# Linear-attention state from five chunks of 115 and 116 rows instead of six of 96, a head's last row by a transfer of its own

## What is computed

```python
kv = einsum('bhsd,bhse->bhde', k, v)          # 8 batches, 8 heads, 576 rows, head size 64
out = einsum('bhsd,bhde->bhse', q, kv)
x = out / sqrt(mean(out * out) + 1e-6) * g_norm     # 4608 x 512
h = x @ w_in;  g = max(h, 0) + alpha * min(h, 0);  y = g @ w_out      # 512 -> 2048 -> 512
e = argmax(y @ w_gate);  out[token] = gate * relu(y @ w1[e]) @ w2[e]  # eight experts
```

## Time and profile before

| | us |
|---|---|
| median of 3 runs | 1503.25 |
| lowest, highest | 1499.38, 1505.24 |
| the profiled execution, its time | 1500.92 |
| the profiled execution, its span | 1499.1 |
| TensorE busy in it | 1468.6 |
| VectorE, ScalarE, GpSimd busy | 723.5, 491.3, 127.6 |

### The profile page before, as it was taken

One profiled execution on the slowest core, in us unless ns is written; L12 is line 12 of the kernel. 1 busy time (PEld: TensorE's weight loads), 2 busy tenths in 40 slices (PEclk: granted clock), 3 DMA queues, 4 the chain that ended last, 5 costly groups with the idle time before them and its releaser, 6 DMA issues.

```text
span 1499.1 us, 27268 instructions
## 1 busy us (share of the span) xinstructions
PE 1468.6 (98%) x8553; PEld 1277.5 (85%) x8554; DVE 723.5 (48%) x1796; ACT 491.3 (33%) x994; POOL 127.6 (9%) x143
## 2 busy tenths in 40 slices
PE   7899999999999999999999999999999999999997
PEld 6788989888898989898989898887888888888886
DVE  3585555565656465645555655663122114444411
ACT  3442232323232323223222221433233234444422
POOL 1000000000000000000000000112111111111111
PEclk8999999999999999999999999999999999999999
DMA  8532121102121102213100000524123114444410
GB/s 193 136 95 70 33 75 33 43 2 75 33 75 33 43 2 61 46 36 71 31 13 23 1 22 1 146 88 156 44 91 106 43 37 149 155 142 157 152 41 32
DMA packets 100516, 104.51 MB, mean 70 GB/s; under 512 B 55296, under 2 KB 75920, under 8 KB 100434
## 3 DMA queue, kind: packets, MB, share of 16 engines
q1 hardware_dynamic: 91618, 80.99, 19.6%
q0 software_dynamic: 7872, 21.09, 4.4%
q10 hardware_dynamic: 944, 1.33, 0.4%
HBM read 84.04 MB, written 20.65 MB: 70 GB/s over the span
## 4 chain that ended last, share of the span: by engine, by line
PE 90%; DMA 4%; DVE 2%; ACT 1%; issue 1%; SPq 1%; POOL 0%; ACTq 0%; POOLq 0%; DVEq 0%
PE psAcc L1346 25%; PE psH L1334 24%; PE psAcc L1469 15%; PE psH L1448 14%; PE psO L1458 2%; PE psO L1279 2%; PE psO L1249 1%; PE psQ L1429 1%; PE psQ L1265 1%; DMA AR<-rows,uid 1%; PE psY L1297 1%; DMA lists<-meta,slot 1%; PE psY L1289 1%; PE psY L1306 1%; DMA AR<-in_v_dram 1%
## 5 line engine op out<-in xcount | busy, mean ns | idle before, releaser
L1346 PE MATMUL psAcc<-W,XG 128*128 128x512 f32 x1728 | 438.9, 399 | 0.0
L1334 PE MATMUL psH<-XG,W 128*128 128x384 f32 x2304 | 436.3, 337 | 2.2 <-DVE W L958 1.4
L1334 PEld LDWEIGHTS psH<-XG,W 128*128 128x128 f32 x2304 | 408.4, 188 | 18.0 <-issue 2.7
L1346 PEld LDWEIGHTS psAcc<-W,XG 128*128 128x128 f32 x1728 | 313.7, 188 | 66.1 <-issue 6.0
L683 ACT ACTIVATE XG<-AR 128x128 fp32r<-128x128 f32 (+1 forms) x384 | 132.1, 364 | 639.9 <-DVE AR L988 634.2
L985 DVE TENSOR_SCALAR AR<-psH,acol 128x384 f32<-128x384 f32 x192 | 118.4, 617 | 296.0 <-PE psH L1334 296.0
L1448 PE MATMUL psH<-W,XG 128*128 (+1 forms) x996 | 250.4, 400 | 0.0
L1469 PE MATMUL psAcc<-W,XG 128*128 (+1 forms) x984 | 243.4, 396 | 0.0
L1469 PEld LDWEIGHTS psAcc<-W,XG 128*128 128x128 f32 x984 | 182.9, 189 | 37.3
L1448 PEld LDWEIGHTS psH<-W,XG 128*128 128x128 f32 x996 | 180.8, 188 | 36.8 <-DVE W L966 0.4
L1153 DVE TENSOR_TENSOR XG<-psO,XG 128x512 fp32r<-128x512 f32 x82 | 56.6, 690 | 222.1 <-ACT XG L742 218.8
(11 more groups left out here) (200 smaller groups left out, 873.3 us busy)
## 6 DMA issues: line engine op xcount, KB each, us to landing
AR<-in_moe_w_dram SPq DMA_DIRECT2D x68, 512.0 KB, 4.9
AR<-in_k_dram SPq DMA_DIRECT2D x16, 576.0 KB, 5.4
rows<-AR SPq DMA_DIRECT2D x36, 256.0 KB, 2.1
AR<-in_q_dram SPq DMA_DIRECT2D x32, 256.0 KB, 3.1
AR<-in_v_dram SPq DMA_DIRECT2D x14, 576.0 KB, 6.8
AR<-in_moe_w_in_dram SPq DMA_DIRECT2D x16, 256.0 KB, 2.9
AR<-in_moe_w_out_dram SPq DMA_DIRECT2D x16, 256.0 KB, 3.5
AR<-in_v_dram ACTq DMA_DIRECT2D x2, 576.0 KB, 9.3
```

What stands on the lines that cost most here:

```text
L1334: mm = pe.matmul(psH[f % 2][:, 0:TILE], w_in_v[:, wp, cc, f * P:(f + 1) * P], xT[:, b, xp, cc, :], start=(cc == 0 and (wp, xp) == PARTS[0] ...
L1346: mm = pe.matmul(psAcc[m][:, :], gT[:, f % 2, gp, m * P:(m + 1) * P], w_out_v[:, wp, f, :], start=(f == 0 and (gp, wp) == PARTS[0]), stop= ...
```

## The change

A head's rows are cut in five chunks instead of six. 576 is 5 x 115 + 1, so partition p, for p from 0 to 114, holds five rows that lie one behind the other (a piece of 1280 bytes), and the last row of each head goes to partition 115, chunk 0, by a transfer of its own with four pieces of 256 bytes. Chunk 0 has 116 rows of contraction, chunks 1 to 4 have 115. Each half then has four transfers instead of two, and `kv_in` counts 64 for a half instead of 32. The areas for k and v shrink from 1536 to 1280 columns each, the unused area becomes `tail_extra`, and `AR` 9984 columns instead of 10240. The areas that lie over each other keep their order.

```diff
-    KVJ = 6
+    KVJ = 5
     KVP = S // KVJ
+    KVR = S - KVJ * KVP
...
-        AR = sb("AR", [P, 2 * KN + 3 * DM + 2 * KN + DM + 3 * DM + DM])
+        AR = sb("AR", [P, 2 * KN + 3 * DM + 3 * DM + DM + 2 * TILE + DM + DM + 4 * DM])
...
-        area(2 * KN - 4 * DM - 2 * TILE)
+        tail_extra = area(DM)
...
         def load_rows(engine, src, b, half, to, signal):
             engine.dma_start(to[0:KVP, :, :, :].rearrange("p h j d -> p h (j d)"),
-                             src[bass.ds(b, 1), half * HH:(half + 1) * HH, :, :].rearrange(
+                             src[bass.ds(b, 1), half * HH:(half + 1) * HH, 0:KVJ * KVP, :].rearrange(
                                  "b h (p j) d -> p (b h) (j d)", j=KVJ)).then_inc(signal, 16)
+            engine.dma_start(to[KVP:KVP + 1, :, 0, :],
+                             src[bass.ds(b, 1), half * HH:(half + 1) * HH, KVJ * KVP:S, :].rearrange(
+                                 "b h s d -> s (b h) d")).then_inc(signal, 16)
...
-                    pe.wait_ge((kv_in, kv_in_1)[n], 32)
+                    pe.wait_ge((kv_in, kv_in_1)[n], 64)
                 else:
-                    pe.wait_ge(kv_in, 32 * n)
+                    pe.wait_ge(kv_in, 64 * n)
...
                     for j in range(KVJ):
+                        n_rows = KVP + (j < KVR)
                         for r in range(2):
-                            mm = pe.matmul(bank[r * D:(r + 1) * D, c * D:(c + 1) * D], kr[0:KVP, 2 * c + r, j, :],
-                                           vr[0:KVP, 2 * c + r, j, :], start=(j == 0), stop=(j == KVJ - 1),
+                            mm = pe.matmul(bank[r * D:(r + 1) * D, c * D:(c + 1) * D], kr[0:n_rows, 2 * c + r, j, :],
+                                           vr[0:n_rows, 2 * c + r, j, :], start=(j == 0), stop=(j == KVJ - 1),
                                            tile_position=(0, r * D))
```

More of the change, by code:

```diff
@@ L64, in attention_dense_moe_routed_moe @@
     LW = 4 * F1
-    assert EARLY == 4 and (B, H, S, D, DM) == (8, 8, 576, 64, 512) and CH * F1 == FC * DM == LW == CH * F2 + FE * DM
+    assert EARLY == 4 and KVR == 1 and (B, H, S, D, DM) == (8, 8, 576, 64, 512) and CH * F1 == FC * DM == LW == CH * F2 + FE * DM
     rows = nc.dram_tensor("rows", (N + 1, DM + META), F32).ap()
@@ L146, in attention_dense_moe_routed_moe @@
                            for m in range(TG - 1)]
-        tail_yT = [yT, qT, AR[:, A2 + 2 * KN - DM:A2 + 2 * KN].rearrange("p (c n) -> p c n", c=CH)]
+        tail_yT = [yT, qT, tail_extra.rearrange("p (c n) -> p c n", c=CH)]
         picked = sb("picked", [P, TG, E], BF16)
```

## The result

| | before | after |
|---|---|---|
| median, us | 1503.46 (5 runs) | 1516.24 (5 runs) |
| lowest, highest | 1499.38, 1506.82 | 1512.91, 1519.26 |
| profiled execution, its time and span | 1500.92, 1499.1 | 1519.26, 1517.4 |

The ratio is 1.0082, with a 95% interval from 1.0066 to 1.0099: the kernel became slower by 12.8 us. The forecast was 1527, in a range from 1508 to 1545.

What follows compares the result with a forecast made beforehand. TensorE, busy 98% of the span and 90% of the chain, was taken as the bound. 18 + 5.3 + 6 - 3.5 = +25.8 on 1500.9 gave 1526.7, 1529 by the median, set at 1527 for overlap; range 1508 to 1545.

Steps and rivals of the forecast that it cites:

- 115 rows are dealt to five engines: Large k and v transfers: equal whole shares of 23 rows let only five engines take part, instead of 16.
- Rival 1: Large transfers: uneven shares, all 16 engines move rows; 1498.9 us, 1501 by the median, not slower; chance 0.12.
- rival 4: Large transfers: all rows on one engine, a pair takes 50 to 80 us, kernel above 1900 us; chance 0.02.
- T: Time for one k and v pair to load on five engines: 14 us, ends 9.9 and 15.9.
- rival 2: Large transfers: five engines, each much faster when the others are idle, pair near 10 us, kernel 1512.5; chance 0.22.
- the case that I held likeliest: Five engines, a pair of loads taking 11.5 to 15.5 us, kernel about 1517 to 1536 us; chance 0.44.
- the same data is the nearest row: Pricing a pair on five engines: the earlier k and v stretch, 79 engine-us, gave 15.9 us, the slow end.
- Start: First two pairs, queued at once: second half starts at 31 instead of 12.97, +18 us (ends +9.7, +21.8).
- Third pair: Pair wanted at 28.07, before the first dense matmul: lands at 33.4, +5.3 us (ends +1.2, +7.2).
- First tile: Fourth pair delays the fifth step's dense weights behind it, from 43.90 to 49.9: +6 us (ends +1.9, +7.9).
- Steady part: Six later pairs of halves: loads of 15.4 us hidden within 25 and 17.1 us, 0; slow end 3.5 us.
- Matmuls: k times v halves: eight fewer records save 0.24 us in each of 14 halves; 3.5 us gained in sum.

## Why the prediction was right, and where it was off

**Direction and mechanism.** The step that decided, "115 rows are dealt to five engines", is shown: by the packet count, which was forecast at about 950 and is 946, by the share of 0.33, and by the cuts at 95, 94, 92 and 90, each of which went with its largest even deal. The two runs that separate the causes are those with 95 and 1 and with 90 and 6: the same number of transfers, the same matmuls, and 0.86% of loss against none. The rule of the Trainium skill (page "DMA: Bandwidth & Descriptors", section "Why a DMA increments its semaphore by 16 and not by 1"), which the trace of before could not show, agrees with every packet count shown here. Rival 1 (uneven shares on 16 engines) and rival 4 (one engine) fall with the same rows.

**The size of T.** The sum took 14 us for a pair, between 9.9 and 15.9. A pair moves in 9.5 us at 124 GB/s, just under the low end (1.18 MB; in the steady pair the first issue is at 165.91, and bytes move until 177.7). This is rival 2, which had a chance of 0.22; the case that I held likeliest, T from 11.5 to 15.5 with a time from 1517 to 1536, did not come. The range held because its low end was drawn for this case. That the first tile's +6, worked out with a T half as long again as the true one, came near the measured +4.7 is luck: at the true T its price was higher than the sum knew. The mistake is in the sentence that the same data is the nearest row. The 99 ns a packet of the earlier trace rows was not the pace of an engine but that of 16 sharing something that gives them 250 to 260 GB/s (what it is, no run shows). With five engines a packet took 58 ns, and 67 ns in the run with 95 rows, whose pieces have the same 1536 bytes (25.3% of 16 engines over 13 us for 786 packets). The row with the better bound was the expert weights' 23.8 GB/s for a busy engine, which two, four and five engines reached (24, 23 and 23 in the table).

**Term by term**, against the low end that belongs to this T:

- Start: +18 was forecast, +9.7 at the low end, +10.1 measured. The chain behind it, from the second half to the first tile's input (the last step of `XG`), takes 17.6 us instead of 17.3, so it kept its length, as assumed. The issues that are held in both queues cost nothing here, as forecast: without the small transfers the second half starts 0.2 us earlier.
- Third pair: +5.3, low end +1.2, measured +1.3 with those 0.3 us of the chain in it (30.34 to 41.75 is 11.4 later). A difference this small is within the spread of the traces; that TensorE waits 1.93 us for this pair, in the trace after itself, is the firmer sign.
- First tile: +6, low end +1.9, measured +4.7. Here the low end was too low, since two things were missing in it. SP is held in the small transfer's issue, which I had costed at nothing on the ground that SP has 25 us between loads; in the first tile it has not, and the next weights are issued 8.0 us after the first dense matmul instead of 6.5. And TensorE's idle stretch of 4.9 us was followed by 4.7 us at a granted clock of 0.50, 1.2 GHz, in which twelve matmuls took 4.18 us instead of 2.33. Counted from the first dense matmul, the 4.7 are 1.5 for the later issue, 2.4 for the weights' longer way from issue to use (9.0 us instead of 6.6), 1.9 for the slow matmuls, and 1.1 given back behind them. The held issue is the case that the prediction named last among its signs of being wrong; here it costs less than the weights' longer way behind the pair.
- Steady part: 0 forecast, none measured (0.9973 against 0.9970); shown by the run with 115 rows from half 4 on.
- Matmuls: 0.24 us a half forecast, 0.23 measured between the two halves of a tile, 2.7 us over the eleven halves from half 4's start to half 15's. Depths of 115, 116 and 128 cost nothing over 96: the halves of the cut at 112 and 16 take the same 1.39 us.

10.1 + 1.3 + 4.7 - 2.9 (the halves from 3 to 14) is the 13.2 us of the table. With T at its low end my sum gave 1512.5; the 2.8 us by which the first tile exceeds its low end bring it to 1515.3, next to 1516.2.

**What I had set aside.** The forecast was drawn down by 2 us for overlap of the start with the third pair. At that place there is none. What overlaps is the late start and the first tile: after a late start the stretch up to half 3 is 2.0 us shorter than before (23.3 for 25.3), and the tile's own pair on five engines makes it 6.7 us longer (30.1). The +4.7 is the difference of the two, so the price of that pair by itself is higher than the term shows.

## What to carry to other kernels

When a cut changes the number of rows of a transfer, factor that number before anything else: what counts is its largest divisor up to 16, and 112 + 16 keeps the gain that 115 + 1 loses. Price such a transfer by the best rate of a busy engine in the trace, not by the mean rate of 16 at once, and ask for each transfer whether it lies in the start, where nothing hides it, or between two uses 17 us apart, where for these 1.18 MB even five engines are enough. A wait of several microseconds on TensorE is to be priced with the slow stretch that can follow it (here twelve matmuls in 4.18 us behind 4.94 of idle time, and in 4.03 behind 7.33).

## What the runs showed that I had not expected

- One engine moves about 25 GB/s (50 with two, 100 with four, 123 with five), and for these pieces the sum stops near 260 with 11 as with 16 (the expert weights reached 392), so the loss grows steep somewhere between 11 engines and five, where no run was made. At 25 GB/s each, ten engines would reach the 250 to 260; that is an estimate from these rows.
- An issue is held behind large transfers of its own queue that are still under way: 8.18 us for a transfer of 1 KB, and q's loads are held if that one is left out (19.13 us for the three). The cost of a small transfer is the place at which it makes its queue wait.
- A chunk of 64 rows between chunks of 128 makes 40 records take 1.82 us instead of 1.39. The Trainium skill, page "TensorEngine Tiling (Array Packing)", section "Tiling Modes", says that a change of the tiling mode drains the array, and lists 64 rows as a mode of its own; the runs agree in that 96 and 120 show nothing, but that the drain is the cause wasn't measured apart.
- With two engines the steady loads stood still for some microseconds between 241 and 245, with SP held in issues. This is open.
